# Half-array products on tile-aligned keys, and probabilities that are divided after the product with the values

## The reference, cut to what matters

```python
k_sum = k.reshape(B, H, nb, block, D).max(axis=3)       # block 32, nb 24
v_sum = v.reshape(B, H, nb, block, D).mean(axis=3)
scores_l = scale * np.matmul(q, k.transpose(0, 1, 3, 2))
mask_l = np.abs(pos[:, None] - pos[None, :]) < window   # window 16
scores_s = scale * np.einsum('bhsd,bhnd->bhsn', q, k_sum) + np.log(block)
scores_all = np.concatenate([np.where(mask_l, scores_l, -1e9), scores_s], axis=-1)
a = np.exp(scores_all - np.max(scores_all, axis=-1, keepdims=True))
a = a / (np.sum(a, axis=-1, keepdims=True) + 1e-09)
out = np.matmul(a, np.concatenate([v, v_sum], axis=2))
```

## Time and profile before

| | us |
|---|---|
| median of 3 runs | 357.35 (356.35 to 358.55) |
| span of the profiled execution | 357.2 |
| first masked scores, last `add_eps` in it | 12.85, 140.40 |
| busy: TensorE, VectorE | 320.7, 233.7 |
| busy: ScalarE, GpSimd | 150.7, 136.4 |

### The profile page before, as it was taken

One profiled execution on the slowest core, in us unless ns is written; L12 is line 12 of the kernel. 1 busy time (PEld: TensorE's weight loads), 2 busy tenths in 40 slices (PEclk: granted clock), 3 DMA queues, 4 the chain that ended last, 5 costly groups with the idle time before them and its releaser, 6 DMA issues.

```text
span 357.2 us, 5495 instructions
## 1 busy us (share of the span) xinstructions
PE 320.7 (90%) x1876; PEld 292.6 (82%) x1876; DVE 233.7 (65%) x638; ACT 150.7 (42%) x416; POOL 136.4 (38%) x118
## 2 busy tenths in 40 slices
PE   8777967775778899996999999999999999999997
PEld 7666856765668788985799999988889999998886
DVE  6799999999999999979888200028886633331000
ACT  3375656664677676363322322243333211112222
POOL 5219367339434212599205700004444933331000
PEclk9899899999999999999899999999999999999999
DMA  8896774266331221233100000011211000001222
GB/s 180 143 212 146 164 167 108 62 157 143 91 87 50 57 67 59 73 119 89 46 0 1 2 0 2 0 44 46 73 30 31 29 2 0 0 2 59 88 109 98
DMA packets 49721, 25.33 MB, mean 71 GB/s; under 512 B 44170, under 2 KB 44446, under 8 KB 49310
## 3 DMA queue, kind: packets, MB, share of 16 engines
q1 hardware_dynamic: 49694, 24.99, 27.7%
HBM read 21.24 MB, written 3.15 MB: 68 GB/s over the span
## 4 chain that ended last, share of the span: by engine, by line
PE 56%; DVE 23%; issue 10%; POOL 5%; DMA 3%; SPq 1%; ACT 1%; DVEq 0%; POOLq 0%
PE psum L592 52%; DVE probs L858 6%; DVE neg_s L839 6%; DVE gate L901 3%; POOL g_lo L458 2%; DMA v_blk<-in_v_dram 2%; DVE sums_eps L847 2%; POOL win_v_lo L458 2%; DVE k_max L871 1%; DVE recip L852 1%; PE psum L675 1%; DVE k_a L880 1%; POOL win_u_lo L458 1%; PE psum L544 1%; DMA raw<-in_moe_w_in_dram 1%
## 5 line engine op out<-in xcount | busy, mean ns | idle before, releaser
L858 DVE TENSOR_SCALAR probs<-probs,recip 128x184 f32<-128x184 f32 x96 | 60.9, 675 | 1.7
L718 ACT ACTIVATE probs<-neg_s,neg_max 128x184 f32<-128x184 f32 x96 | 42.2, 441 | 44.8 <-DVE neg_max L839 44.5
L458 POOL TENSOR_TENSOR g_lo<-work,g_hi 128x384 fp32r<-128x384 f32 x32 | 36.3, 1147 | 46.8 <-ACT g_hi L819 25.8
L544 PE MATMUL psum<-ident,probs 128*128 128x128 f32 x144 | 25.8, 288 | 22.4 <-DVE probs L858 22.1
L901 DVE SCALAR_TENSOR_TENSOR gate<-xT,conv_c,gate 128x384 f32<-128x384 f32 (+8 forms) x44 | 41.7, 956 | 1.3
L544 PEld LDWEIGHTS psum<-ident,probs 128*128 128x128 f32 x144 | 16.0, 143 | 29.4 <-DVE probs L858 28.7
L458 POOL TENSOR_TENSOR vn_lo<-work,vn_hi 128x512 fp32r<-128x512 f32 x12 | 15.5, 1293 | 57.2 <-DVE vn_hi L1040 57.2
L839 DVE CUSTOM_DVE_ANT_0 neg_s<-psum,mask 128x184 f32<-128x184 f32 x96 | 29.2, 340 | 0.0
L1018 DVE TENSOR_TENSOR wsp_lo<-psum,wsp_hi 128x384 fp32r<-128x384 f32 x12 | 6.6, 548 | 33.6 <-ACT wsp_hi L800 33.6
L458 POOL TENSOR_TENSOR x_lo<-xT,x_hi 128x768 fp32r<-128x768 f32 x8 | 15.0, 1869 | 32.2 <-DVE x_hi L863 32.2
L1050 DVE TENSOR_TENSOR work<-psum,b_row 128x384 f32<-128x384 f32 x16 | 8.9, 558 | 27.8 <-PE psum L592 26.2
(11 more groups left out here) (125 smaller groups left out, 791.3 us busy)
## 6 DMA issues: line engine op xcount, KB each, us to landing
k_nat<-in_k_dram SPq DMA_DIRECT2D x16, 192.0 KB, 3.2
q_nat<-in_q_dram SPq DMA_DIRECT2D x16, 192.0 KB, 3.3
v_blk<-in_v_dram SPq DMA_DIRECT2D x4, 768.0 KB, 7.6
out_dram<-work SPq DMA_DIRECT2D x11, 256.0 KB, 2.0
v_main<-in_v_dram SPq DMA_DIRECT2D x16, 160.0 KB
raw<-in_moe_w_spatial_dram SPq DMA_DIRECT2D x6, 384.0 KB, 3.0
raw<-in_moe_w_out_dram SPq DMA_DIRECT2D x8, 256.0 KB, 2.7
raw<-in_moe_w_in_dram SPq DMA_DIRECT2D x8, 256.0 KB, 2.9
```

Of the source, the lines that this page charges most:

```text
L458: nc.gpsimd.tensor_tensor(dst_lo, src, dst_hi.bitcast(F32), ALU.subtract).then_inc(lo_sem, 1)
L544: ins = nc.tensor.transpose(bank_t(i)[:, n * P:(n + 1) * P], probs[:, i % 4, c:c + P], ident[:, :])
L718: ins = nc.scalar.activation(probs[:, i % 4, w], neg_s[:, i % 3, w], ACT.Exp, bias=neg_max[:, i % 4, h:h + 1], scale=-1.0, accum_out=sums[ ...
L858: ins = nc.vector.tensor_scalar(a, a, recip[:, i % 4, h:h + 1], None, ALU.mult)
```

## The change

Keys are stored once, in `k_win`, per tile as [tails and block maxima | 128 main keys | tails and block maxima] = 56 + 128 + 56 columns. Head b's window is the first 184 columns, head a's the last 184, and each score product reads only its head's 64 partitions (half of the array's rows) and writes a bank of its own; the score banks are 0 to 2 in turn, the turned probabilities have bank 3 alone. `k_heads` becomes `k_tails`, two small copies. The product with the values becomes two of 64 output partitions each, on unshifted values `v_nat`, and one full one on `v_rest` (112 rows). The pass `normalise` is gone: `turn_probs` waits for the exponentials alone. `invert_sums` now writes the reciprocal of each head's sum over 64 columns (128x128 in all), TensorE turns that (`spread_recip`), and after ScalarE has copied the undivided result, VectorE multiplies it in (`scale_x`). Loads of values per pair go from 10 to 8.

```diff
-    WIN = P + 2 * WINDOW
-    HEAD = WIN + NB
+    SIDE = 2 * WINDOW + NB
+    HEAD, SC, WIDE = P + SIDE, 2 * (P + SIDE), P + 2 * SIDE
+    MAIN, LEFT, RIGHT, SUMS = SIDE, 0, WINDOW, 2 * WINDOW
+    KEYS = (slice(MAIN, WIDE), slice(0, HEAD))
+    MAIN_A, REST, MAIN_B = 0, P, P + 2 * SIDE
...
-        def bank_s(i):
-            return psum[:, i % 2, :]
-        def bank_t(i):
-            return psum[:, 2 + i % 2, :]
+        def bank_s(i, h):
+            return psum[:, (2 * i + h) % 3, 0:HEAD]
+        bank_t = psum[:, 3, 0:3 * P]
...
-                nc.gpsimd.tensor_tensor(k_a[:, s, :, 0:WIN], windows(kT), own[:, 0:1].broadcast_to((P, T, WIN)),
-                                        ALU.mult)
-                nc.gpsimd.tensor_tensor(k_b[:, s, :], kT[:, :], own[:, 1:2].broadcast_to((P, S + 2 * WINDOW)),
-                                        ALU.mult).then_inc(k_heads_ready, 1)
+                nc.gpsimd.tensor_copy(sides(p, 1, T - 1, LEFT, WINDOW),
+                                      twice(k_win[:, s, 0:T - 1, MAIN + P - WINDOW:MAIN + P]))
+                nc.gpsimd.tensor_copy(sides(p, 0, T - 1, RIGHT, WINDOW),
+                                      twice(k_win[:, s, 1:T, MAIN:MAIN + WINDOW])).then_inc(k_tails_ready, 1)
...
-                if i >= 2:
-                    pe.wait_ge(masked, i - 1)
-                lhs = qT[:, s, t * P:(t + 1) * P]
-                o = bank_s(i)
-                nc.tensor.matmul(o[:, 0:WIN_B], lhs, k_a[:, s, t, :], start=True, stop=True)
-                nc.tensor.matmul(o[:, WIN_B:SC], lhs, k_b[:, s, t * P:t * P + WIN], start=True,
-                                 stop=True).then_inc(scores_ready, 1)
+                if i >= 1:
+                    pe.wait_ge(masked, 2 * i - 1)
+                for h in range(2):
+                    d = slice(h * D, (h + 1) * D)
+                    ins = nc.tensor.matmul(bank_s(i, h), qT[d, s, t * P:(t + 1) * P], k_win[d, s, t, KEYS[h]],
+                                           start=True, stop=True)
+                ins.then_inc(scores_ready, 1)
 
             def turn_probs(i):
-                pe.wait_ge(probs_ready, i + 1)
-                if i >= 2:
-                    pe.wait_ge(probsT_ready, i - 1)
+                pe.wait_ge(exp_done, i + 1)
+                if i >= 1:
+                    pe.wait_ge(probsT_ready, i)
...
-                nc.tensor.matmul(o, v_main[:, s, t, 0:P], pT[:, 0:P], start=True, stop=False)
-                nc.tensor.matmul(o, v_main[:, s, t, D:D + P], pT[:, P:2 * P], start=False, stop=False)
-                nc.tensor.matmul(o, v_rest[:, s, t, :], pT[:, 2 * P:3 * P], start=False,
-                                 stop=True).then_inc(x_summed, 1)
+                nc.tensor.matmul(o[0:D], v_nat[:, s, t, 0:D], pT[:, 0:P], start=True, stop=False,
+                                 skip_group_check=True)
+                nc.tensor.matmul(o[D:P], v_nat[:, s, t, D:P], pT[:, P:2 * P], start=True, stop=False,
+                                 skip_group_check=True)
+                nc.tensor.matmul(o, v_rest[0:2 * SIDE, s, t, :], pT[0:2 * SIDE, 2 * P:3 * P], start=False, stop=True,
+                                 skip_group_check=True).then_inc(x_summed, 1)
+
+            def spread_recip(i):
+                pe.wait_ge(recip_ready, i + 1)
+                n = 2 * P + i % 2 * P
+                nc.tensor.transpose(bank_x(i)[:, n:n + P], recip[:, i % 4, :], ident[:, :]).then_inc(spread_done, 1)
...
-                act.wait_ge(x_summed, 2 * j + 2)
+                act.wait_ge(spread_done, 2 * j + 2)
                 p, r = divmod(2 * j, T)
                 nc.scalar.activation(xT[:, p, r * P:(r + 2) * P], bank_x(2 * j)[:, 0:2 * P],
-                                     ACT.Copy).then_inc(xT_ready, 1)
+                                     ACT.Copy).then_inc(x_taken, 1)
...
             def invert_sums(i):
                 dve.wait_ge(eps_added, i + 1)
-                nc.vector.reciprocal(recip[:, i % 4, :], sums_eps[:, i % 4, :]).then_inc(recip_ready, 1)
-
-            def normalise(i):
-                dve.wait_ge(recip_ready, i + 1)
-                for h in range(2):
-                    a = probs[:, i % 4, h * HEAD:(h + 1) * HEAD]
-                    ins = nc.vector.tensor_scalar(a, a, recip[:, i % 4, h:h + 1], None, ALU.mult)
-                ins.then_inc(probs_ready, 1)
+                if i >= 4:
+                    dve.wait_ge(spread_done, i - 3)
+                nc.vector.reciprocal(recip[:, i % 4, :].rearrange("p (h d) -> p h d", d=D),
+                                     sums_eps[:, i % 4, :].rearrange("p (h d) -> p h d", d=1).broadcast_to(
+                                         (P, 2, D))).then_inc(recip_ready, 1)
+
+            def scale_x(j):
+                dve.wait_ge(x_taken, j + 1)
+                p, r = divmod(2 * j, T)
+                x = xT[:, p, r * P:(r + 2) * P]
+                nc.vector.tensor_tensor(x, x, bank_x(2 * j)[:, 2 * P:4 * P], ALU.mult).then_inc(xT_ready, 1)
...
-                for h, n in enumerate((SUM_A, SUM_B)):
-                    ins = nc.vector.tensor_scalar(k_a[:, p % 2, :, n:n + NB],
-                                                  k_max[:, :].rearrange("p (a n) -> p a n", a=1).broadcast_to(
-                                                      (P, T, NB)), own[:, h:h + 1], None, ALU.mult)
+                sums_of = k_max[:, :].rearrange("p (a n) -> p a n", a=1)
+                ins = nc.vector.tensor_copy(sides(p, 0, T, SUMS, NB), twice(sums_of.broadcast_to((P, T, NB))))
...
-            for i in range(STEPS + 2):
+            for i in range(STEPS + 6):
                 p, t = divmod(i, T)
-                if i >= 2:
-                    normalise(i - 2)
+                if i >= 7 and i % 2 == 1:
+                    scale_x((i - 7) // 2)
```

More of the change, by code:

```diff
@@ L100, in attention_gated_mlp @@
             qT = sb("qT", [P, 2, S], F32, att)
-            v_main = sb("v_main", [P, 2, T, 3 * D], F32, att)
+            v_nat = sb("v_nat", [P, 2, T, P], F32, att)
         wu_hi = sb("wu_hi", [P, C, DM], F32R)
@@ L404, in link, with keep, k_tails @@
                     pool.wait_ge(mask_step, n)
+                def keep(x, base, down, step):
+                    pattern = [[0, n] for n in x.shape[1:-1]] + [[step, x.shape[-1]]]
+                    link(nc.gpsimd.affine_select(out=x, in_=x, compare_op=ALU.is_ge, fill=OUTSIDE, base=base,
+                                                 pattern=pattern, channel_multiplier=down))
                 link(nc.gpsimd.memset(mask[:, 1, :], 0.0))
-                for w in (0, WIN_B):
-                    m = mask[:, 1, w:w + WIN]
-                    link(nc.gpsimd.affine_select(out=m, in_=m, compare_op=ALU.is_ge, fill=OUTSIDE, base=-1,
-                                                 pattern=[[1, WIN]], channel_multiplier=-1))
-                    link(nc.gpsimd.affine_select(out=m, in_=m, compare_op=ALU.is_ge, fill=OUTSIDE,
-                                                 base=2 * WINDOW - 1, pattern=[[-1, WIN]],
-                                                 channel_multiplier=1))
-                link(nc.gpsimd.memset(mask[:, 1, SUM_A:WIN_B], LN_BLOCK * float(D) ** 0.5))
-            def k_heads(p):
+                main = mask[:, 1, MAIN:MAIN + P]
+                keep(main, WINDOW - 1, -1, 1)
+                keep(main, WINDOW - 1, 1, -1)
+                for o in (0, HEAD):
+                    keep(mask[:, 1, o + LEFT:o + LEFT + WINDOW], -1, -1, 1)
+                    keep(mask[:, 1, o + RIGHT:o + RIGHT + WINDOW], WINDOW - P - 1, 1, -1)
+                    link(nc.gpsimd.memset(mask[:, 1, o + SUMS:o + SIDE], LN_BLOCK * float(D) ** 0.5))
+            def k_tails(p):
                 pool.wait_ge(kT_ready, p + 1)
@@ L752, in _ @@
             turned_k(0)
-            turned(0, qT[:, 0, :], q_turned, qT_ready)
+            turned_q(0)
             act.wait_ge(conv_turned, 1)
@@ L768, in _ @@
                 if t == 3 and p + 1 < PAIRS:
-                    turned(p + 1, qT[:, (p + 1) % 2, :], q_turned, qT_ready)
+                    turned_q(p + 1)
                 if t == 3 and 1 <= p <= W_OUT:
@@ L911, in _ @@
             nc.vector.memset(v_rest[:, :, :, :], 0.0).then_inc(v_zeros, 1)
-            nc.vector.memset(v_main[:, :, :, :], 0.0).then_inc(v_zeros, 1)
             dve.wait_ge(mask_step, MASK_STEPS)
@@ L917, in _ @@
             dve.wait_ge(edge_step, 2)
-            for w in (0, WIN_B):
-                nc.vector.memset(mask[:, 0, w:w + WINDOW], OUTSIDE)
-                ins = nc.vector.memset(mask[:, 2, w + WIN - WINDOW:w + WIN], OUTSIDE)
+            for n in (0, HEAD):
+                nc.vector.memset(mask[:, 0, n + LEFT:n + LEFT + WINDOW], OUTSIDE)
+                ins = nc.vector.memset(mask[:, 2, n + RIGHT:n + RIGHT + WINDOW], OUTSIDE)
             ins.then_inc(edge_step, 1)
             dve.wait_ge(edge_step, 3)
-            dve.wait_ge(pool_zeros, 4)
             max_k(0, (0, 1))
             sum_k(0)
```

(12 more changed lines are left out.)

128 lines of the change are left out of this document (56 added, 72 removed).

## The result

The kernel before took 357.38 us (356.35 to 358.55), the changed one 350.12 us (median of 346.03, 348.39, 351.84 and 353.10). The forecast was 351, range 333 to 364, and "faster" at 0.55.

What follows compares the result with a forecast made beforehand. VectorE was taken to bound the attention; -57 + 33.6 + 8.2 - 1 + 4 + 6 = -6.2 us on 357.2 gave 351 us, range 333 to 364.

Steps and rivals of the forecast that it cites:

- Part 1: VectorE in the attention: `normalise` goes, taking 57 us off.
- part 5: VectorE standing behind GpSimd: 23 us of GpSimd key products leave, remaining standing adds 4 us, mainly at epsilon.
- Part 2: VectorE's reciprocal grows from 2 to 128 columns at 6.4 ns a column: +33.6 us over 48.
- Rivals A and B: Wide reciprocal: A, fast as any other operation, 335 us, chance 0.20; B, 8.2 ns a column, 362 us, chance 0.22.
- Part 3: VectorE's new `scale_x`, 24 times on 128x256 with one operand in PSUM: +8.2 us.
- part 4: VectorE: `sum_k` becomes one copy, first key product and memset of `v_main` go: about -1 us.
- Part 6: New VectorE waits, for ScalarE's copy before `scale_x` and TensorE's pace in steps without an extra: +6 us.
- Part 7: TensorE's step becomes 1.95 us, under VectorE's 2.5, so it does not bind and halves gain nothing.
- rival C: TensorE bounds through four changes of array shape a step, 0.17 us each: 358 us, chance 0.13.
- The sign set for C: TensorE's distance from last score product to first turn: 0.11 us, not 0.3, tells against rival C.
- Part 8: Loads: two fewer small ones per pair, in a stage where none is a chain piece: 0 us.

Runs made afterwards that it cites:

- division_only: The kernel before with the new division alone, on its full-array products and old GpSimd key products: 360.19 us, ratio 1.0075.
- warm: The changed kernel with 22 turns of the identity on TensorE behind the first scores: 348.10 us, ratio 0.9713.
- late_scale: The changed kernel with `scale_x` moved from ahead of the masks to behind them in the same iteration: 349.83 us, ratio 0.9818.
- the last kernel: The changed kernel without epsilon, `scale_x` behind the masks, 22 identity turns, a two-column reciprocal widened by ScalarE: 335.68 us, ratio 0.9386.
- wide_no_eps_warm: The changed kernel, its reciprocal still wide, without epsilon, with `scale_x` behind the masks and 22 identity turns: 338.73 us, ratio 0.9497.
- halves_busy_pool: The changed kernel with the old division, plus two idle GpSimd products ahead of each pair's small key copies: 362.82 us, ratio 1.0109.
- the 330.9 us: The 335.68 us kernel on full-array products and shifted windows, GpSimd's key products of pairs 1 to 7 cut (keys not the reference's): 330.88 us, ratio 0.9257.
- halves_only: The changed kernel with the old division put back, keeping the new keys, scores and values: 343.27 us, ratio 0.9587.

## Why the prediction was right, point by point

- **Part 1** held as a sum and failed as a reading. "Most of the passes that stood behind GpSimd are gone with part 1" (part 5) is refuted by `division_only`: of the 31 us as much as 22.8 came back in other lines. They go only when GpSimd's products go too. The -57 is the gain of both halves of the change together, and I had booked it all to the division. In the attention's stretch the division is +3.6 by itself, the key layout -12.8 by itself, and the division on top of the layout +6.5, since `normalise` has by then only 45.2 us to give back; by the ratios of the whole kernels the three are +2.7, -14.8 and +4.3. The signs agree, the sizes carry the clock.
- **Part 2** held: 943 ns against 0.95 forecast, 0.86 from start to start against 0.89. From two columns (156) to 128 that is 6.2 ns a column. Rivals A and B fall with it. The estimate behind it rested on 12 ns between two instructions of one trace, so that it hit so closely is in part luck. Of the rule on the Trainium skill's page "VectorE: DVE Perf Modes", section "First, the fixed hardware budget", a divide repeated 8 times, the trace bears out the direction and not the 8.2 ns.
- **Part 3** (7.5 us against 8.2) and **part 4** (0.7 against 1) held.
- **Part 5** held in size (+4.3 against +4) for the changed kernel, with epsilon as the main carrier as forecast. It was undervalued as a place to look: epsilon took 12.2 us from start to start and about 6 of the attention hang on it at equal clock, as much as the whole change brought there.
- **Part 6** agrees in its total, 7.4 us of waits against 6, and by luck. The wait for ScalarE's copy is 4.0. The other 3.4 were to be TensorE's pace in steps without an extra, and all of them lie in the stretches at 1.2 GHz, which the prediction did not foresee; in `warm`, without the first of these, they are 0.6, and the copy's 1.6. Removing the wait for the copy gave nothing (`late_scale`).
- **Part 7** held, at full clock, where it said that TensorE does not bind and that the halves earn nothing in this kernel. Its sizes were off. The scores of two half-array products take 0.51 to 0.52 us and not 0.62, and the two halves of the values do run beside each other:

```profile
128.44 0.27 PE L527 MATMUL psum<-ident,probs 128*112 128x128 f32 x1
128.64 0.32 PE L543 MATMUL psum<-probsT,v_nat 128*64 128x128 f32 x1
128.65 0.32 PE L545 MATMUL psum<-probsT,v_nat 128*64 128x128 f32 x1
128.80 0.27 PE L543 MATMUL psum<-probsT,v_nat 128*64 128x128 f32 x1
```

  They start 0.01 apart, as the first half of the rule on the Trainium skill's page "TensorEngine Tiling (Array Packing)", section "Tiling Modes", has it, and a change of shape does cost time, as its second half has it: 0.20 from the last turn to the first half where instructions of one shape follow 0.11 apart, so 0.1 and not rival C's 0.17. C's place was right and its price too high for this kernel. The sign set for C, 0.11 or 0.3 us from the last score instruction to the first turn, read 0.25:

```profile
79.95 0.32 PE L517 MATMUL psum<-k_win,qT 64*128 64x184 f32 x2
80.20 0.33 PE L525 MATMUL psum<-ident,probs 128*128 128x128 f32 x1
```

  The 0.11 was set too low: 184 columns take about 0.16 by themselves, an estimate between the 0.14 of 160 columns and the 0.18 of 208 in full arrays. That leaves 0.09 for the change of shape, once more about half of C's price.
- **Part 8**: nothing seen. Behind the attention: 210.13 us both times, as forecast within 1 us.
- **Not foreseen: the clock in the attention.** The changed kernel has TensorE at 1.2 GHz for 27 us in the profiled execution, 17 of them from 12.5 on; before, it was 10. Its four executions had spans of 344.2, 346.6, 350.0 and 351.3 us at mean clocks of 0.975, 0.966, 0.961 and 0.947: the lower the clock, the longer, over the whole 7 us of their spread. At 1.2 GHz a step of TensorE takes 3.32 us (22.50 to 25.82), longer than VectorE's, and VectorE stands for it:

```profile
22.50 0.99 PE L517 MATMUL psum<-k_win,qT 64*128 64x184 f32 x4
25.82 0.99 PE L517 MATMUL psum<-k_win,qT 64*128 64x184 f32 x4
```

So the time was right for a sum whose largest terms were right, with luck in part 6 and none booked for the clock, which in `warm` was worth some 3 us of the attention; and the reason in front of it was half wrong: the change is a good layout of the keys and a division that does not pay as long as epsilon stands where it does.

**Open.** How much of the last kernel's gain over `wide_no_eps_warm` (3 us, on different chips) is ScalarE's widening was not measured on one chip. `halves_busy_pool` mixes the standing, the low clock and keys that come later. Whether the 330.9 us can be had with the keys of both heads really made, by an engine other than GpSimd, wasn't tried. Why the granted clock falls in the middle of the attention in some kernels and not in others (at 84 us in the changed one, at 60 in `halves_only`) was followed in one place only.

## What to carry to other kernels

Before crediting a removed VectorE pass with its busy time, split that time into work and standing behind GpSimd: here some three quarters of the standing stayed in the kernel and moved to the passes that were left, however short, until GpSimd's own work was cut. In a loop that VectorE bounds, the cheapest edits are then less work for GpSimd and fewer short passes. A wide reciprocal is dear (0.86 us a step here), but to widen afterwards is not shown to pay: the copy on VectorE, which can stand itself, gained nothing by the ratios, and for that on ScalarE the intervals overlap. On TensorE count each change of array shape as 0.1 us before using half arrays.

## What the runs showed of the hardware

- A float32 reciprocal costs 6.2 ns a column (943 ns for 128, 156 for two), six times the 1.02 ns of the plain slope, and does not stand behind GpSimd: the longest of 48 took 953 ns, and 17 of them ran beside a GpSimd instruction. An addition on two columns does stand, up to 2015 ns.
- With 22 turns of the identity (2.62 us) where TensorE had been idle, its granted clock was 1.00 (2.4 GHz) from 12 to 30 us, where the same kernel without them had 0.53.
- Two half-array products with 64 output columns each start 0.01 us apart, and a change of array shape adds about 0.1 us (0.20 where 0.11 is the distance within one shape).
